# Thresholded attention beside two MLPs: the normalisation moved to VectorE, the last PV tile uncut, fewer idle matmuls

## What is computed

```python
scores = scale * q @ k.T                                   # 576 x 576 for each batch and head
thresh = max(scores, axis=-1) - tau                        # tau = 0.02
scores = where(scores >= thresh, scores, -1e9)
attn = exp(scores - max(scores, axis=-1))
attn = attn / (sum(attn, axis=-1) + 1e-09)
x = (attn @ v) laid out as 2304 x 512
h = x @ w_in1;  g = h * sigmoid(1.702 * h);      x = g @ w_out1    # 512 -> 2048 -> 512
h = x @ w_in2;  g = h * tanh(softplus(h));       out = g @ w_out2
```

## Time and profile before

| | us |
|---|---|
| median of three runs | 1143.89 (1142.0 to 1144.36) |
| the profiled execution | 1142.0 |
| its span, first to last instruction | 1140.2 |
| busy PE / PEld | 1118.2 / 997.6 |
| busy DVE / ACT / POOL | 665.4 / 703.8 / 260.7 |

### The profile page before, as it was taken

One profiled execution on the slowest core, in us unless ns is written; L12 is line 12 of the kernel. 1 busy time (PEld: TensorE's weight loads), 2 busy tenths in 40 slices (PEclk: granted clock), 3 DMA queues, 4 the chain that ended last, 5 costly groups with the idle time before them and its releaser, 6 DMA issues.

```text
span 1140.2 us, 19451 instructions
## 1 busy us (share of the span) xinstructions
PE 1118.2 (98%) x7638; PEld 997.6 (87%) x7638; DVE 665.4 (58%) x1231; ACT 703.8 (62%) x939; POOL 260.7 (23%) x446
## 2 busy tenths in 40 slices
PE   9899999999999999999999999999999999999998
PEld 6578778989888989888988999998989989998997
DVE  4777777667667767777765334675443345344333
ACT  4688887676777776777775222585554464455453
POOL 3566753333334333333431000000000000000000
PEclk9999999999999999999999999999999999999999
DMA  2544432222332232332220105410000000000000
GB/s 63 160 145 144 132 115 89 77 78 72 87 106 78 72 104 62 91 91 82 74 82 21 41 20 167 139 56 28 28 28 1 28 28 29 29 28 28 1 28 28
DMA packets 60156, 78.73 MB, mean 69 GB/s; under 512 B 6561, under 2 KB 45985, under 8 KB 60065
## 3 DMA queue, kind: packets, MB, share of 16 engines
q1 hardware_dynamic: 60064, 77.49, 22.5%
HBM read 63.83 MB, written 13.63 MB: 68 GB/s over the span
## 4 chain that ended last, share of the span: by engine, by line
PE 87%; ACT 6%; DVE 4%; issue 2%; POOL 0%; ACTq 0%; POOLq 0%; DVEq 0%
PE ps_s L727 18%; PE ps_r L612 15%; PE ps_r L632 14%; PE ps_r L750 9%; PE ps_t L481 7%; PE ps_s L463 6%; PE ps_t L504 5%; PE ps_t L750 5%; PE ps_t L632 4%; PE ps_r L497 2%; PE ps_t L507 2%; ACT e_buf L514 1%; PE ps_s L452 1%; PE ps_t L612 1%; DVE x_lo L783 1%
## 5 line engine op out<-in xcount | busy, mean ns | idle before, releaser
L550 DVE SCALAR_TENSOR_TENSOR e_buf<-ps_s,neg_thr,e_buf 128x576 f32<-128x576 f32 x144 | 117.6, 817 | 91.9 <-ACT e_buf L514 86.4
L612 PE MATMUL ps_r<-x_hi,wi_lo 128*128 128x256 f32 x544 | 157.8, 290 | 0.1
L612 PE MATMUL ps_r<-x_lo,wi_hi 128*128 128x256 f32 x544 | 153.6, 282 | 0.0
L612 PE MATMUL ps_r<-x_hi,wi_hi 128*128 128x256 f32 x544 | 153.5, 282 | 0.0
L794 DVE COPY hidden<-ps_s 128x768 f32<-128x768 f32 x48 | 45.9, 957 | 170.5 <-PE ps_s L727 170.5
L823 ACT ACTIVATE m_lo_raw<-m_lo_raw 128x1536 f32<-128x1536 f32 x24 | 35.8, 1492 | 168.7 <-DVE m_lo_raw L801 168.7
L526 ACT COPY pt<-ps_t 128x640 f32<-128x640 f32 x144 | 100.0, 694 | 63.8 <-PE ps_t L481 61.6
L632 PE MATMUL ps_r<-g_hi,wo_lo 128*128 128x256 f32 x464 | 135.4, 292 | 0.0
L727 PE MATMUL ps_s<-x_hi,wi_lo 128*128 128x384 f32 x384 | 129.0, 336 | 2.4 <-DVE x_lo L783 2.4
L578 POOL TENSOR_SCALAR neg_thr<-neg_max,tau_sb 128x1 f32<-128x1 f32 x144 | 68.4, 475 | 273.3 <-DVE neg_max L543 273.3
L632 PE MATMUL ps_r<-g_lo,wo_hi 128*128 128x256 f32 x464 | 130.9, 282 | 0.0
(11 more groups left out here) (100 smaller groups left out, 2697.4 us busy)
## 6 DMA issues: line engine op xcount, KB each, us to landing
k_ll_raw<-in_k SPq DMA_DIRECT2D x56, 288.0 KB, 2.8
v_raw<-in_v SPq DMA_DIRECT2D x64, 160.0 KB, 2.2
wi_lo_raw<-in_moe_w_in SPq DMA_DIRECT2D x16, 512.0 KB, 3.9
wo_lo_raw<-in_moe_w_out SPq DMA_DIRECT2D x16, 512.0 KB, 4.1
q_raw<-in_q SPq DMA_DIRECT2D x32, 192.0 KB, 3.0
x_scratch<-y_acc SPq DMA_DIRECT2D x9, 512.0 KB, 3.5
x_lo_raw<-x_scratch SPq DMA_DIRECT2D x6, 768.0 KB, 4.8
out_rows<-rows_out SPq DMA_DIRECT2D x18, 256.0 KB, 2.1
```

The source lines that it names most:

```text
L550: dve.scalar_tensor_tensor(out=e, in0=scores(n), scalar=neg_thr[:, c], in1=e, op0=ALU.is_le, op1=ALU.mult, accum_out=row_sum[:, c]).then_i ...
L612: mm = pe.matmul(bank[:, part * CH:(part + 1) * CH], wi[w][:, k, f * P:(f + 1) * P], x[:, k, :], start=t == 0, stop=t == 3 * KT - 1)
```

## The change

The cut of the last tile of a later group goes: every tile is one product of full height and width, alternating between the two sides, so that three tiles fall to the first side and two to the second. The normalisation of steps 16 to 143 goes from ACT to DVE, where it stands behind the reciprocal of its step and ahead of the pieces, the sum of the group and the next maximum; it is one tensor_scalar with two per-partition scalars. The first idle matmuls become six instead of nine, those of slot 0 three instead of six.

```diff
-            bank, v, moving = pv_bank(g), v_raw[u % 2], pv_moving(g)
-            if g < H:
-                for j in range(NJ):
-                    mm = pe.matmul(bank[0:D, 0:w], v[:, j, :], moving[:, j, :], start=j == 0, stop=j == NJ - 1)
-                mm.then_inc(s["pv_done"], 1)
-                return
-            sides = (slice(0, D), slice(D, P))
-            for j in range(NJ - 1):
-                pe.matmul(bank[sides[j % 2], 0:w], v[:, j, :], moving[:, j, :], start=j < 2, stop=False)
-            for side in range(2):
-                c = slice(side * w // 2, (side + 1) * w // 2)
-                mm = pe.matmul(bank[sides[side], c], v[0:D, NJ - 1, :], moving[0:D, NJ - 1, c], start=False, stop=True)
+            sides = 1 if g < H else 2
+            for j in range(NJ):
+                rows = slice((j % sides) * D, (j % sides + 1) * D)
+                mm = pe.matmul(pv_bank(g)[rows, 0:w], v_raw[u % 2][:, j, :], pv_moving(g)[:, j, :],
+                               start=j < sides, stop=j >= NJ - sides)
             mm.then_inc(s["pv_done"], 1)
...
-        def act_norm(act, n):
+        def dve_norm(dve, n):
             e = e_buf[n % 3][:, 0:S]
-            act.wait_ge(s["inverted"], n + 1)
-            act.wait_ge(s["share_ready"], n + 1)
-            act.activation(e, e, ACT.Identity, bias=even_share[:, n % 4:n % 4 + 1],
-                           scale=inv_sum[:, n % 4:n % 4 + 1]).then_inc(s["normed"], 1)
+            dve.wait_ge(s["inverted"], n + 1)
+            dve.wait_ge(s["share_ready"], n + 1)
+            dve.tensor_scalar(e, e, inv_sum[:, n % 4:n % 4 + 1], even_share[:, n % 4:n % 4 + 1], ALU.mult,
+                              ALU.add).then_inc(s["normed"], 1)
...
-            pe_idle(pe, 9)
+            pe_idle(pe, 6)
             pe_scores(pe, 0)
...
                     if n < 5:
-                        pe_idle(pe, 6 if n == 0 else 3)
+                        pe_idle(pe, 3)
...
-                    if n - 1 >= FRONT:
-                        act_norm(act, n - 1)
                     if n >= 0:
                         act_exp(act, n)
...
-                    if n - 1 < N:
-                        act_norm(act, n - 1)
...
                     dve_mask(dve, n - 1)
                     dve_inv(dve, n - 1)
+                    if n - 1 >= FRONT:
+                        dve_norm(dve, n - 1)
```

## The result

The changed kernel took 1157.43 us at the median of four executions (1157.38 to 1162.58), the kernel before 1142.95 beside it. The ratio is 1.0148 with an interval of 1.0122 to 1.0174: 14.5 us slower, where the prediction had 2.8. The sign was right and the size was not, and the time lies 4.4 us above the range. Ten executions of it are on record in all: four at 1157.4 to 1157.5, two at 1161.1 and four at 1162.4 to 1162.8. The profiled one is one of the longest, 1162.4 us around a span of 1160.6.

What follows compares the result with a forecast made beforehand. PE, busy 98% of the span, was taken as the bound. Terms 5.2 - 6.7 + 5.0 - 0.7 = +2.8 us gave 1144.8 us for the profiled execution, 1146.7 on the median's scale; range 1141.5 to 1153.

Steps and rivals of the forecast that it cites:

- PV products, +5.2: PE's PV products in 56 later groups: six pass steps per group without the cut tile, +5.2 us.
- ACT gives back, -6.7: ACT without the 0.87 us normalisation: PE waits less for x_pair, and three other stalls go, -6.7 us.
- DVE pays, +5.0: Normalisation on DVE: PE waits where DVE lacks idle time or POOL holds it, +5.0 us, bounds 0.5 and 8.
- 0.46 us vanishes: DVE ahead of x_pair: in 51 of 56 groups its idle time, 0.93 us each, hides the 0.46 us normalisation.
- The exchange: Moving the normalisation from ACT to DVE, what ACT gives back and DVE pays together: -1.7 us.
- The hold itself: POOL's weight subtractions hold DVE's normalisation in eleven of steps 19 to 38; five reach PE, 3.6 us.
- 0.46 us for one: Length of one normalisation of 576 elements on DVE, taken at the clip's rate: 0.46 us.
- Fewer idle matmuls, -0.7: Start of the kernel: first exponential at 6.93 us instead of 7.63, -0.7 us, between 0 and -1.2.
- the clock falls back: Rival, chance 0.05: PE idle ahead of the third scores goes on at 1.2 GHz, +6 us over three steps, 1152.
- DVE the bound: Rival, chance 0.08: at 0.77 us per normalisation sixteen close pairs of groups run late, +10 us more, 1156.

Runs made afterwards that it cites:

- experiment 2: Kernel before with only the last PV tile left uncut, so whole PV products: 1147.59 us, ratio 1.0035.
- 11: Kernel after with the normalisation behind the next step's maximum and idle matmuls back at nine and six: 1146.17 us, ratio 1.0026 to the kernel before.
- experiment 5: Kernel before with only the normalisation moved to DVE, queued behind the next step's maximum: 1141.76 us, ratio 0.9983.
- experiment 3: Kernel before with only the normalisation moved to DVE as in the change, ahead of the maximum: 1156.43 us, ratio 1.0117.
- experiments 6 to 8: Normalisation on DVE only from step 40: 1148.44 us; low weight parts left out, with normalisation on DVE: 1147.03 us, on ACT: 1142.22 us; each against the kernel before.
- experiment 1: Kernel before with only the idle matmuls reduced, six at the start and three in slot 0: 1143.34 us, ratio 1.0002.

## Why the prediction was wrong

- **PV products, +5.2.** The mechanism and the size per group were right: 322.51 to 324.27 is 1.76 us and 332.59 to 334.03 is 1.44, as forecast, and the other groups of the trace agree. That a group now changes the mode of the array once less did not make it shorter. Over 32 and 24 groups it is 5.0 us. On the end 3.5 to 3.8 arrived (experiments 2 and 11), so some 1.3 us vanish in waits that PE had anyway. The timeline of the kernel after:

```profile
322.51 1.83 PE L499 MATMUL ps_t<-pt,v_raw 128*64 128x320 f32 x10
324.27 0.66 PE L481 MATMUL ps_t<-ident,e_buf 128*128 128x128 f32 x4
...
332.59 1.51 PE L499 MATMUL ps_t<-pt,v_raw 128*64 128x256 f32 x10
334.03 0.66 PE L481 MATMUL ps_t<-ident,e_buf 128*128 128x128 f32 x4
```

- **ACT gives back, -6.7.** This step failed. It took ACT as the late one at a dozen groups and let ACT's 0.87 us come off. ACT could not use it: its exponential waits for the maximum, and that had just been put behind the normalisation (13.0 us of such waits before, 74.3 after). Such waits need not cost anything by themselves (47.6 us of them are left in experiment 5); what PE pays for is x_pair behind them. Where the place is right (experiment 5) the 4.2 us that I counted at x_pair do come, as 4.5, but PE and its loader wait 3.2 us for the normalisation instead of 1.9, and now and then for queries and gated pieces that stand behind it. The end shows 1 to 2 us. Two of the stalls counted beside x_pair, at 92.60 and 72.99: the first is 0.39 us long there instead of 0.70, the second is gone, though its row names issue and not the mask that I had it wait for.
- **DVE pays, +5.0.** The failed step is its form: "0.46 us vanishes" in the idle time ahead of x_pair. I priced the operation by who waits for x_pair and left out who waits for the maximum, which is in every step. The exchange was forecast at -1.7 us and measured at +12.3 (experiment 3). About 8 us of it come with the holds, falls of the clock included, and 4 to 5 are the normal operation ahead of the maximum (experiments 6 to 8). Both vanish when it moves behind the maximum (experiment 5), the holds in part because there are fewer of them.
- **The hold itself** was right in mechanism, and in size for one: 1.35 us against 0.58, at ten of the steps 19 to 38 where I had eleven (nine of 1.32 to 1.36 us and the one of 1.66). POOL's key subtractions mostly have 0.16 us left and cost nothing; one, at step 18, has 0.44 left, and there the normalisation lasts 0.75. The page SBUF — State Buffer of the Trainium skill, Who interferes with whom, says that whoever issues first holds the shared ports for the whole instruction, and that a reduction on DVE never contends. The traces agree: in the kernel after the seven maxima that run beside a POOL subtraction last 745 ns in the mean and those with none 748. In experiment 5 the normalisation mostly starts ahead of POOL's threshold, and it is the threshold that lengthens, from 489 to 605 ns. The recorded starts are not exact enough to tell the order at 150.28: there the normalisation is listed 0.08 us ahead of the subtraction that it was held by. Only the price on the end was off: I let five holds count 0.7 us each, and all ten counted, with a fall of the clock on top.
- **0.46 us for one.** Measured 0.58. The term was mis-sized by 0.12 us. If the clip of the earlier trace rows has the same rate, the fixed part is larger than the 0.16 us that I took from two rows of unlike kind; no run parts rate and fixed part. This shifts less than the place does: behind the maximum 0.58 us is free.
- **Fewer idle matmuls, -0.7.** The lowest execution of experiment 1 is 0.7 us under before's, as forecast; six lie at 1142.7 to 1143.6 with a fall of the clock, under before's like ones near 1144.2. In the other five of 12 the time lies where a rise some 15 us later puts it, at a cost of 4.7, as in the trace. I had this as a rival, "the clock falls back", with 0.05 and +6 us. The price was near, by another way than I gave: PE was not idle ahead of the third scores and did not fall back, it had not risen yet (first exponential at 7.56 us, not 6.9). The chance was far too low. The page TensorE: Matmul & The Clock Gate of the Trainium skill, Part 1, says that what a kernel loses at its start varies from run to run. The sets of executions here agree: the two sets of experiment 1, one and the same kernel, have medians 3.9 us apart.
- **DVE the bound** gave 1156 with 0.08, nearest to what came, but by the wrong way: 0.77 us each and close pairs of groups. DVE is not the bound in total. At 83 of 100 us busy, experiment 5 is as quick as the kernel before.

What stays open: which executions rise late at the start, since they occur with every count of idle matmuls; why a fall of the clock follows a standstill of PE in one execution and not in another; and what a hold costs behind the maximum.

## What to carry to other kernels

When an operation moves to another engine, don't price it by that engine's busy share or its idle time at one consumer: list what is queued behind it on the engine it goes to, and who waits for that. The idle time that hides an operation is the one at its own place in the queue, so the first thing to try is the place behind the result that others wait for. An engine that is given time back uses it only if its inputs come earlier too.

## What the runs showed of the hardware

- A standstill of PE of about 2 us can cost more than itself: after 1.93 us at 55.7 us (experiment 2) and 2.06 us at 150.9 us (the kernel after) the granted clock was 0.50 for some 3 us and the passes took double time, 1.6 us lost each. It does not always: the first of these waits is in thirteen traces, and a fall follows in five. With six idle matmuls in it the granted clock was 1.000 in eleven executions of eleven.
- At the start the lower pace lasted to between 17 and 21 us in five traces and to between 5 and 7 us in nine, and PE's rows stand without a gap between them from 1.5 us on in the late ones. The clock row of the profile says 1.00 all the while, since the trace has no record of the clock there; the distance between matmuls is the witness.
- The hold between POOL and DVE works in both directions: a normalisation of 0.58 us that starts 0.26 us into a POOL subtraction lasts 1.35, and one that starts ahead of POOL's threshold lengthens that, from 489 to 605 ns in the mean of all. A maximum on DVE beside a POOL subtraction is not lengthened (745 ns against 748).
